# A delta-rule recurrence ahead of two expert layers: the recurrence's operand layout, gate products, order of work and prologue are rewritten

## The reference

```python
# q, k, v: 4 batches x 8 heads x 768 steps x 48
k_n = k / (norm(k) + 1e-6)
for t in range(S):
    y[t] = q[t] @ state
    state += beta[t] * outer(k_n[t], v[t] - k_n[t] @ state)
x = y as 3072 tokens of 384
e = argmax(x @ w_gate); gate_w = softmax(x @ w_gate)[e]; eom = sigmoid(x @ w_output_gate)[e]
x = gate_w * eom * (relu(x @ w1[e]) @ w2[e])                   # 8 experts, F = 1024
out = sum over 4 experts of p[:, e] * (relu(x @ v1[e]) @ v2[e])
```

## Time and profile before

| | us |
|---|---|
| Median of 3 runs (lowest 1657.09, highest 1664.24) | 1657.15 |
| The profiled execution | 1644.96 |
| Its span, first to last instruction | 1643.1 |
| TensorE busy in the span | 1498.3 |
| VectorE, ScalarE (ACT), GpSimd (POOL) busy | 685.0, 293.2, 256.9 |
| Mean granted clock of TensorE | 0.90 of full |

### The profile page before, as it was taken

How to read it: one execution, slowest core, us unless ns; L and a number is a source line. 1 busy time by engine, 2 the same in 40 slices (tenths; PEclk the granted TensorE clock), 3 DMA queues, 4 the chain that set the end, 5 groups by cost and what they waited for, 6 DMA issues and landing times.

```text
span 1643.1 us, 37079 instructions
## 1 busy us (share of the span) xinstructions
PE 1498.3 (91%) x14930; PEld 1454.7 (89%) x14931; DVE 685.0 (42%) x1457; ACT 293.2 (18%) x639; POOL 256.9 (16%) x134
## 2 busy tenths in 40 slices
PE   4399999999907999999789999999999999999998
PEld 4399899999806888889689999999999999999998
DVE  3555665564144555555444323333332332333232
ACT  3021222221130112110043211111111111111111
POOL 2000100100065334530033200202002020020000
PEclk8575887687658999999889999999999999999999
DMA  8224334322063333511231110100001010000022
GB/s 162 44 60 96 72 76 100 83 47 68 2 251 127 115 118 117 167 67 38 79 109 39 42 36 0 39 0 29 10 0 38 0 38 0 0 0 0 14 47 54
DMA packets 103804, 97.98 MB, mean 60 GB/s; under 512 B 59936, under 2 KB 91040, under 8 KB 102560
## 3 DMA queue, kind: packets, MB, share of 16 engines
q1 hardware_dynamic: 89120, 62.00, 15.4%
q10 hardware_dynamic: 11520, 25.17, 4.6%
q0 software_dynamic: 3072, 9.44, 1.7%
HBM read 71.41 MB, written 25.17 MB: 59 GB/s over the span
## 4 chain that ended last, share of the span: by engine, by line
PE 85%; issue 7%; DVE 3%; DMA 2%; ACT 1%; SPq 1%; POOL 0%; DVEq 0%; ACTq 0%
PE bank L632 22%; PE bank L634 21%; PE bank L633 21%; PE bank L462 14%; PE bank L663 1%; PE bank L560 1%; PE bank L563 1%; PE bank L578 1%; DVE terms L932 1%; DVE inverse L936 1%; PE bank L639 1%; ACT R L759 1%; PE bank L572 1%; DMA y_sorted<-y_sb 1%; SPq L296 0%
## 5 line engine op out<-in xcount | busy, mean ns | idle before, releaser
L632 PE MATMUL bank<-x2Th,v1h 128*128 (+1 forms) x768 | 257.4, 335 | 3.6 <-issue 3.6
L632 PE MATMUL bank<-v2h,gTh 128*128 128x384 f32 x768 | 258.5, 337 | 0.0
L633 PE MATMUL bank<-x2Tl,v1h 128*128 (+1 forms) x768 | 257.1, 335 | 0.0
L634 PE MATMUL bank<-x2Th,v1l 128*128 (+1 forms) x768 | 257.1, 335 | 0.0
L634 PE MATMUL bank<-v2h,gTl 128*128 128x384 f32 x768 | 256.8, 334 | 0.0
L633 PE MATMUL bank<-v2l,gTh 128*128 128x384 f32 x768 | 256.6, 334 | 0.0
L1186 DVE SCALAR_TENSOR_TENSOR gTl<-bank,gTh 128x384 fp32r<-128x384 f32 x256 | 142.7, 558 | 269.8 <-ACT gTh L870 268.4
L870 ACT ACTIVATE gTh<-bank 128x384 fp32r<-128x384 f32 x256 | 126.1, 492 | 637.2 <-PE bank L634 626.5
L1195 DVE SCALAR_TENSOR_TENSOR x_all<-bank,p_sb,x_all 128x384 f32 (+1 forms) x192 | 106.7, 612 | 259.0 <-PE bank L634 259.0
L632 PEld LDWEIGHTS bank<-x2Th,v1h 128*128 128x128 f32 x768 | 144.7, 188 | 4.0 <-issue 4.0
L633 PEld LDWEIGHTS bank<-x2Tl,v1h 128*128 128x128 f32 x768 | 144.7, 188 | 0.0
(11 more groups left out here) (156 smaller groups left out, 2118.3 us busy)
## 6 DMA issues: line engine op xcount, KB each, us to landing
w_raw<-in_moe_w_dram ACTq DMA_DIRECT2D x16, 1536.0 KB, 6.9
v_raw<-in_moe_w_dram SPq DMA_DIRECT2D x16, 768.0 KB, 4.4
kq_sb<-in_kq_dram SPq DMA_DIRECT2D x24, 384.0 KB, 7.6
x_sorted<-zeros SPq DMA_DIRECT2D x11, 576.0 KB, 4.1
xs_in<-x_sorted SPq DMA_DIRECT2D x33, 192.0 KB, 2.3
y_sorted<-y_sb SPq DMA_DIRECT2D x31, 192.0 KB, 1.9
kt_sb<-in_kt_dram SPq DMA_DIRECT2D x12, 392.0 KB, 7.8
vt_sb<-in_vt_dram SPq DMA_DIRECT2D x12, 384.0 KB, 8.1
```

The costliest lines, as they stand in the source:

```text
L632: pe.matmul(dst, lh, rh, start=first, stop=False)
L633: pe.matmul(dst, lh, rl, start=False, stop=False)
L634: return pe.matmul(dst, ll, rh, start=False, stop=last)
```

## The change

Only the recurrence changes.

1. Keys and queries are padded with zero rows to 64 in each half, so all products of the recurrence use 64 rows.
2. The gate products take the 16 gate columns as the weights, and xT_gate of both halves (256 columns) moves; the 16x256 result is copied and transposed back. One chain per chunk serves both halves. The transposes use bank 5 and 6 after read_out's result has been copied.
3. R is scaled by -gain, and signs in the levels change with it.
4. Substitution works on the two 8x8 diagonal blocks of each 16x16 block together (7 columns), and join_left and join_right (two operations of 512 elements each) fill the corner.
5. The lists of TensorE, ACT and VectorE in an iteration are in another order. In chunk 0 the products with the state, which is zero, are left out.
6. Prologue: kq of chunk 0 is loaded by ACT's queue, VectorE scales the second half of gram 0, half of the block DMAs of chunk 0 go by ACT's queue, products and substitution are in another order, and keep_warm issues products whose result isn't used: 10 at the start, 20 before the levels of chunk 0.

The diff, cut to these:

```diff
-                    sp.dma_start(kq_sb[HALVES[a]:HALVES[a] + D, n % NKQ], kq[n, a]).then_inc(kq_in[n % NKQ], 16)
+                    sp.dma_start(kq_sb[HALVES[a]:HALVES[a] + CH, n % NKQ], kq[n, a]).then_inc(kq_in[n % NKQ], 16)
...
+            def keep_warm(count):
+                for _ in range(count):
+                    mul(bank[7][:, 0:128], ones[:], ones[:])
...
+            def gates_product(c):
+                pe.wait_ge(xt_ok, 2 * c + 2)
...
+                for m in range(KD):
+                    last = pe.matmul(bank[7][0:2 * NE, 0:NP * 128], wg[:, m, :], xT_gate[:, m].rearrange("q p n -> q (p n)"),
+                                     start=(m == 0), stop=(m == KD - 1))
+                last.then_inc(lt_mm, 1)
...
             for c in range(NC):
...
+                if ahead:
                     gram_product(c + 3, 0)
-                    query_product(c + 3, 0)
                 solve(c, 0)
                 solve(c, 1)
-                if c + 3 < NC:
-                    gram_product(c + 3, 1)
-                    query_product(c + 3, 1)
-                if c + 1 < NC:
+                if c >= 1:
+                    gates_turned(c - 1)
+                if onward:
                     advance(c, 0)
                     advance(c, 1)
                     level16_left(c + 1)
+                if ahead:
+                    query_product(c + 3, 0)
                 read_out(c, 0)
...
                     level16_right(c + 1)
+                if c >= 1:
+                    gates_product(c - 1)
                 read_out(c, 1)
-                if c >= 1:
-                    gates_turned(c - 1, 0)
-                if c + 1 < NC:
+                if ahead:
+                    gram_product(c + 3, 1)
+                if onward:
                     level32_left(c + 1)
                 if c >= 1:
-                    gates_product(c - 1, 0)
-                    gates_turned(c - 1, 1)
-                if c + 1 < NC:
+                    gates_back(c - 1)
+                if ahead:
+                    query_product(c + 3, 1)
+                if onward:
                     level32_right(c + 1)
...
+            def first_in():
+                act.wait_ge(inverse_out, 16)
+                act.wait_ge(y_clear, 1)
+                for u in range(NU // 2):
...
+                    act.dma_start(Y[rows, 0, :, cols], inverse_blocks[0, u].rearrange("h j i -> j h i")).then_inc(y0_in[0], 16)
...
+            def join_left(n):
+                T, G = whole_block(inverse, n), whole_block(gram, n)
+                shape = [128, HB, HB, HB]
+                dve.tensor_tensor(terms[:], T[:, 0:HB, 0:HB].unsqueeze(2).to_broadcast(shape),
+                                  G[:, 0:HB, HB:BS].rearrange("p k b -> p b k").unsqueeze(1).to_broadcast(shape), ALU.mult)\
+                   .then_inc(sub_chain, 1)
```

More of the change, by code:

```diff
@@ L119, in fused_kernel @@
         state = place("state", [128, 2, NPAIR, D])
-        xT_gate = place("xT_gate", [128, KD, 128])
-        gram = place("gram", [128, 2, BS, BS])
-        inverse = place("inverse", [128, 2, BS, BS])
-        terms = place("terms", [128, BS, BS])
+        xT_gate = place("xT_gate", [128, KD, NP, 128])
+        logits_T = place("logits_T", [2 * NE, NP, 128])
+        HB = BS // 2
+        PITCH = HB * BS + HB
+        gram = place("gram", [128, 2, 2 * PITCH])
+        inverse = place("inverse", [128, 2, 2 * PITCH])
+        terms = place("terms", [128, HB, HB, HB])
+        corner = place("corner", [128, HB, HB])
         assert cursor[0] <= nc.sbuf_usable_end, (cursor[0], nc.sbuf_usable_end)
@@ L277, in blocks_out @@
                 sp.wait_ge(r_ok, 2 * n + 2)
-                for u in range(NU):
+                for u in range(NU // 2 if n == 0 else 0, NU):
                     rows, cols = slice(BS * u, BS * u + BS), slice(BS * (u % 4), BS * (u % 4) + BS)
@@ L379, in _ @@
         def _(pool):
-            for n in range(NY):
-                pool.memset(Y[:, n], 0.0).then_inc(y_clear, 1)
             pool.memset(inverse[:], 0.0).then_inc(cleared, 1)
@@ L556, in read_out @@
                 if c >= 1:
-                    pe.wait_ge(x_ok, 2 * c + p - 1)
+                    pe.wait_ge(xt_ok, 2 * c + p - 1)
                 for h in heads(p):
-                    for a in HALVES:
-                        pe.matmul(bank[5 + p][half_rows(a), small(p, h)], kq_sb[half_rows(a, D), c % NKQ, h, CH:2 * CH],
-                                  state[half_rows(a, D), c % 2, h], start=True, stop=False)
+                    if c >= 1:
+                        for a in HALVES:
+                            pe.matmul(bank[5 + p][half_rows(a), small(p, h)], kq_sb[half_rows(a), c % NKQ, h, CH:2 * CH],
+                                      state[half_rows(a), c % 2, h], start=True, stop=False)
@@ L575, in gates_product, with gates_turned @@
-            def gates_product(c, p):
-                pe.wait_ge(xt_ok, 2 * c + p + 1)
-                for m in range(KD):
-                    last = pe.matmul(bank[7][:, 0:2 * NE], xT_gate[:, m, :], wg[:, m, :], start=(m == 0), stop=(m == KD - 1))
-                last.then_inc(lg_mm, 1)
-            for n in range(3):
-                for p in range(NP):
-                    gram_product(n, p)
-                    query_product(n, p)
+            def gates_turned(c):
+                for p in range(NP):
+                    pe.wait_ge(x_ok, 2 * c + p + 1)
+                    for m in range(KD):
+                        last = pe.transpose(bank[5 + p][:, 128 * m:128 * m + 128], x_all[:, NP * c + p, 128 * m:128 * m + 128], ident)
+                last.then_inc(xt_mm, 1)
@@ new lines, in _ @@
+            pe.wait_ge(ones_ok, 1)
+            keep_warm(10)
+            gram_product(0, 0)
+            gram_product(0, 1)
+            query_product(0, 0)
+            gram_product(1, 0)
+            query_product(0, 1)
+            gram_product(1, 1)
+            query_product(1, 0)
+            gram_product(2, 0)
+            query_product(1, 1)
+            gram_product(2, 1)
+            query_product(2, 0)
+            query_product(2, 1)
+            pe.wait_ge(substituted, 1)
+            keep_warm(20)
@@ L991, in _ @@
             query_masked(0, 1)
+            key_lengths(1)
+            dve.wait_ge(eye_ok, 1)
+            for i in range(1, HB):
+                substitute(0, i)
+            join_left(0)
+            join_right(0)
             squares_summed(2)
@@ L995, in _ @@
             query_masked(1, 1)
+            for i in range(1, HB):
+                substitute(1, i)
+            query_masked(2, 0)
+            blocks_turned(0)
+            join_left(1)
+            join_right(1)
             squares_summed(3)
+            level16_taken(0)
+            query_masked(2, 1)
             key_lengths(3)
[L998 to L1006 removed]
             level32_taken(0)
[L1008 removed]
             for c in range(NC):
[L1010 to L1017 removed]
+                ahead, onward, deep = c + 3 < NC, c + 1 < NC, c + 2 < NC
+                if c >= 1:
+                    error_taken(c, 0)
+                    error_taken(c, 1)
+                if onward:
                     blocks_turned(c + 1)
```

258 lines of the change are left out of this document (149 added, 109 removed).

## The result

The kernel after takes 1662.88 us (median of 20 runs, 1655.98 to 1670.27); the kernel before, in 20 runs beside it, 1658.51 (1635.60 to 1664.24). The ratio is 1.0051 with a 95% interval of 1.0028 to 1.0075: slower by half a per cent, with the whole interval above 1. The profiled execution took 1661.27 us (span 1659.5), against 1644.96 (span 1643.1) before.

A forecast was written before the change was run, and what follows sets the result against it. TensorE was taken to bound the recurrence, at a granted clock of 0.74 of 2.4 GHz. Terms of -12 - 1 + 34 - 3 - 6 = +12 us on a base of 1653 gave 1665 us, range 1622 to 1695.

The forecast's parts named there:

- the prediction's last part: Expected trace: transpose waits for Y 7 us or more, TensorE idle before advance, clock low at advance, high before second gram.
- the ring: Per chunk: transpose, delta, advance to second gram (behind second read_out), scaling, SP's gram and inverse DMAs, next transpose; 36.2 us against 32.0.
- the first rival: Recurrence: Y comes before VectorE asks, TensorE bounds at the high clock; 25.6 us a chunk, 1580 us; chance 0.09.
- Step 4: SP and DMA, from the late scaling through gram load, inverse out and Y to the transpose: 13.8 us, bounds 12.9 and 16.3.
- step 2: TensorE from advance to the late gram: 384 records and gate product, low clock 10.3 us after a stall, 17.75 us.
- The second rival: Same DMA wait but clock high: advance to late gram 12.9 us, a chunk 31.3, 1626 us; chance 0.11.
- The third rival: Clock low until the late gram, not back behind query product and first read_out: 43.1 us a chunk, 1720; chance 0.10.
- 64-row keys: nothing on TensorE: Recurrence products: 48-row and 64-row products cost the same, 238 and 237 ns, so no change on TensorE.
- Substitution: 6.2: VectorE, 8x8 blocks: 6.2 us a chunk against 8.7; nothing in the loop, 2.5 us for each bare in the prologue.
- Gate products: TensorE: six 256-column records, 1.6 us a chunk at the high level, as before; no gain and no loss.
- Prologue and end: First delta at 82.5 against 94.74, -12 us; chunks 9 to 11 -3; from delta 11 to the gates' first reduction -6.
- The base: Whole kernel before taken as 1653 us, between its profiled execution of 1644.96 and median of 1657.15.

The follow-up runs named there:

- the run with the steps exchanged: Kernel after, SP sends the inverse of chunk c+2 out and into Y before the gram blocks of chunk c+3: 1586.2 us, ratio 0.9545.
- the run with 42 products: Kernel after, 42 unused products put on TensorE between gate transposes and advance in chunks 1 to 9: 1657.11 us, ratio 0.9991.
- the exchanged kernel before: Kernel before, SP sends the inverse of chunk c+2 out and into Y before the gram blocks of chunk c+3: 1703.38 us, ratio 1.0233.
- 30 products: Kernel after, 30 unused products put on TensorE between gate transposes and advance in chunks 1 to 9: 1667.37 us, ratio 1.0065.
- the early gram: Kernel after, second gram product back directly behind solve on TensorE, its scaling directly behind the first on ACT: 1590.24 us, ratio 0.9562.

## Why the prediction was right, and where its steps were off

**The mechanism: right, and shown from both ends.** The wait for Y became the largest of the recurrence, TensorE stands idle between the gate transposes and advance, the clock is low when advance runs and high ahead of the late gram, as the prediction's last part asked. Opening the ring at SP's order or at the gram's place takes 73 to 77 us away, close to what the first rival gave for no ring (1580, a chunk of 25.6; measured 1586 and 27.8 at a clock of 0.91).

**The ring's sum, 36.2 us: measured 36.8, with two errors that offset each other in part.** From delta to the late scaling the sum had 18.7 (0.55 + 0.1 + 17.75 + 0.3); in chunks 1 to 8 it is 18.1 on the mean, one chunk with 15.3 in which the clock rose 4 us behind delta, the others between 18.1 and 18.95. The scaling is 1.75 as said, the transpose to delta 2.0 (1.2 in the last two). Step 4 was mis-sized: 13.8, measured 15.1 (14.0 to 16.2). Part of it is one term: the inverse on its way out, up to the next issue, takes 250.04 - 246.65 = 3.4 us in the chunk shown and 2.1 to 3.5 in the others, where I had 1.7 from the earlier trace rows. There it went alone; here it stands right behind the gram load. In the run with the steps exchanged it goes alone again:

```profile
176.55 0.33 SPq L299 DMA_DIRECT2D inverse_blocks<-inverse  x1
178.26 5.54 SPq L305 DMA_DIRECT2D Y<-inverse_blocks  x8
```

1.71 us. With eight chunks the ring gave +38.4 in place of +34. The stall that I put at 7 us is 9.0 (TensorE's wait for delta is 72.1 us in the eight chunks).

**The clock in step 2: right in size.** The high-clock variant was 13.9 from delta to the scaling (0.55 + 0.1 + 12.9 + 0.3), the run with 42 products shows 13.9, 14.7 and 14.9 in its three chunks with the high clock and no pause. The second rival's chunk of 31.3 came out at 31.8 in the best of them. The third rival's point held as well: the clock came back at 230.40, during the first read_out (228.35 to 231.14).

**"64-row keys: nothing on TensorE": wrong.** The price of one product is indeed the same, but the step left out what rows do to the clock. I took 10.3 us of low clock from a kernel with 48 rows and put it behind a stall of a kernel with 64. It came out near (11.2), but with 48 rows in this order of work it would have been 20.0, and a chunk 40.6. The term was right by luck.

**Substitution: 6.2, measured 6.9 in the prologue** (37.90 to 44.84): the two multiplications of 512 elements take 1.01 and 1.02 us (L1020, L1030), not the 0.68 of the mask, and the two sums 0.69 each (L1024, L1034). Nothing hung on it in the loop, as predicted.

**Gate products: right.** 1.6 us a chunk predicted; 11.8 us in eight chunks:

```profile
L595 PE MATMUL bank<-xT_gate,wg 128*16 128x256 f32 x48 | 11.8, 381 | 0.0
```

**Prologue and end.** The first delta at 81.12 (predicted 82.5): the gram load left at 35.8 instead of 38.6, the transpose came at 57.27 instead of 61, and the levels took longer (62.87 to 78.28) as the clock fell in the second one (15.4 us in place of 14). -13.6 for -12. Chunks 9 to 11 gave +0.7 in place of -3: the last ring is 28.6 (27.6 said), and the chunk behind it 22.7 instead of 19.5, as it doesn't run at the high clock throughout (0.73 over both). The end gave -8.9 for -6, since all of it is at the high clock.

**The base.** The sum gave +12 on the profiled execution, and +16.3 is what the two profiled executions show. That the forecast of 1665.0 lies 2 us from the measured 1662.9 is luck, and owed to the base: I let the kernel before be 8 us above its own profiled run at 1653 and added 12; over 20 runs its median is 13.5 above, and that of after 1.6 above its own. The range of before's runs is 29 us wide, of after's 14. In the trace of before two of the eight chunks took 39.0 and 37.8 us, with the clock low from 125.5 to 163.0 and from 296.0 to 323.5, the others 25.9 to 31.2; how many of such chunks a run has would explain its spread. That is argued from one trace, not shown.

## What to carry to other kernels

Where one queue serves several stages in a fixed order, a product that is moved later on one engine holds everything behind it in that queue: follow each moved release to the list that waits for it, and see what stands next there. If the sum shows a ring, open it at the cheapest place before anything else is tuned; here it was the order of two steps, worth 77 us to a rewrite that gave nothing without it. And try such an exchange in the kernel that it is meant for: the same lines cost the kernel before some 40 us (47 by the medians, 39 by the ratio).

## What the runs showed of the hardware

The price of a product and its effect on the clock are two things: 48 and 64 rows take the same time, and with 48 the low stretch behind a stall was 20.0 us and with 64 11.2, TensorE busy in both.

TensorE's pauses without a releaser are waits for its own instructions. The profile has a DMA queue for them, q8; here it is beside TensorE's records, between two pauses of the run with SP's steps exchanged:

```profile
172.49:288.16 115.67, 107.89 (x2928) 100.11 (x2927) 72.23 (x167) 31.56 (x105) 9.46 (x8) 0.90 0.46 108
```

```profile
q8 instruction: 23, 0.38, 1.5%
```

That is one packet of 16.5 KB for each 127.3 matmul records and as many weight loads. All runs together have 47 pauses of 1 us or more between 80 and 440 us (without the eight in which a level waited for X's transpose), 1.2 to 4.5 us long. From one pause of a run to the next there are 509 to 2926 matmul records, and each of these 37 distances is a multiple of 127.3, to within 3 records: the pauses fall where one packet's instructions end, wherever in a chunk that is. Ahead of every one a packet of q8 stands 2.2 to 3.0 us before TensorE goes on, and at least 6 us behind the packet before it. With the exchange alone the packets come 3.5 to 3.8 us apart at the high clock where no load is in the way (175.0, 178.8, 182.3, 186.0). In the exchanged kernel before there is one at 279.0 and none for the next ten us, while the DMA engines are full; these are the queues from 279.5 to 289.5 and from 289.5 to 290.0 (packets, MB, share of the 16 engines):

```profile
q1 hardware_dynamic: 897, 2.15, 88.1%
```

```profile
q1 hardware_dynamic: 50, 0.13, 65.7%
q8 instruction: 1, 0.02, 13.5%
```

TensorE stops at 289.77 and goes on at 292.46. The Trainium skill (Runtime: NRT & Kernel Launch, Instruction fetch mechanics) says that an engine's instructions come in blocks of 16 KiB, 256 instructions, over a DMA queue of its own, and that this is mostly hidden. The block agrees with these packets (16.5 KB, 254.6 records of matmuls and weight loads); for most packets it is hidden here too, and for these 47 it is not. That the packet is late because of the loads is read from the rows; moving the loads alone was not tried. The kernel after has no such pause in its chunks: its loads leave SP at the end of the stall (254.34), and the work behind it is at the low clock. The three variants with its full stall (30 products, 48 rows, no products in the prologue) have none either. So the ring seems to have hidden these pauses as well.

The clock and these pauses go together. It is low within 3 us of the end of 40 of the 47 pauses, and was high ahead of nearly all of them. With the early gram it falls seven times between 108 and 343 us, each time within a pause or less than 2 us behind it, and stays low for 3.5 to 14 us; with 42 products in the stall it falls four times in the eight chunks, each time at one of the five pauses. In that run the five chunks with a pause brought the late scaling 16.7 to 23.1 us behind delta, and the three without one 13.9 to 14.9. There are falls without a pause (the exchange alone, at 304.5, where TensorE had waited 1.7 us for delta) and pauses without a fall: the kernel before pauses for 1.75 us up to 201.32 and the clock stays high. That a pause makes the clock fall is therefore likely and not shown. What is left to gain in the kernels without the ring may be the place of the loads.
